# Attention outputs of two heads in the column halves of the array, and the first layer's input rows in that order

## The chip, the core and the metric
The kernel runs as one program on one core of a Trainium2 chip. The metric is the device time of one execution in microseconds (us). TensorE (PE) multiplies, and its weight loads are listed apart (PEld); VectorE (DVE), ScalarE (ACT) and GpSimd (POOL) do elementwise work; SyncE (SP) only issues transfers, and ScalarE issues some too. The engines run their own instruction streams in order and meet at semaphores.

## The reference
Three steps, in float32:

```
S[t] = a[t] * S[t-1] + k[t] v[t]^T      (a complex, |a| clipped to 0.999; batch 4, 8 heads, 768 steps, head size 48)
y[t] = q[t] . Re S[t]                   -> x: 3072 rows (batch x time) of 384 (heads x 48)
h = x @ w_in;  x2 = (h * clip(h + 3, 0, 6) / 6) @ w_out        (384 -> 2048 -> 384)
h = x2 @ w_in2; out = (max(h, 0) + alpha * min(h, 0)) @ w_out2 (384 -> 2048 -> 384)
```

## The kernel before
**Attention.** Time is cut into 24 chunks of 128 steps (six per batch). For a chunk, VectorE and ScalarE work out decay and phase of all heads (square root, arctangent, sine on ScalarE; reciprocals, running products and sums on VectorE), and multiply them into q and k (`prod`). Transfers from SyncE (`stack`, lines 328 to 338) and ScalarE (line 505) stack real and imaginary part of each head on 96 partitions (`st`). TensorE then forms the scores of four heads at a time (`score`, line 959), transposes k (`turn_k`, 968), and after VectorE's causal mask (719) the outputs (`outputs`, 971 to 984) and the new state (`new_state`, 990). These matmuls are in plain float32, each shown as two records. A batch's first chunk has no state yet, its last makes none.

**Outputs before.** The 384 rows of x are heads x 48, and they must lie on 3 blocks of 128 partitions. A head crosses a block's edge twice, so `head_tiles` lists 10 (head, block) pairs. Each is one matmul with 128 output columns, whose weights are a window of a zero-padded v (`v_pad`, 1536 columns) that puts the head's 48 columns at the right place; 10 more with `s_pad` add the state's part. ScalarE copies the result rounded (`x_high`, 516) and VectorE the rest (`x_low`, 725) into `x_hi` and `x_lo`.

**The two layers.** 8 units of 384 rows of x (three chunks each), 16 items a unit, 128 items a layer. An item is `hidden(n)`: 9 matmuls of 384 columns in float32r (three row blocks, each high x high, high x low, low x high), a gate on ScalarE and VectorE, a split into two parts (ScalarE line 528, POOL 439), and `output(n)`: 9 more. `output(n)` and `hidden(n + 3)` follow each other on TensorE.

**The order.** It is written out in `places()`. Slots run from -3 to 24; slots 0, 1, 2 have chunks 0, 1, 2, slot 3 has none, slots 4 to 24 have chunks 3 to 23. Each slot has positions 0 to 4 or more, one item to a position. While chunk c0 is at the scores, c1 and c2, the two behind it, are prepared on VectorE and ScalarE. TensorE does scores at position 0, outputs and state at 1; VectorE does `phases` and `mask` at 0, the products at 1, `x_low` and the state at 2, reciprocals at 3 and 4. SyncE's queue at position 2: the stacking of c1 (six transfers, then two), the loads of `a` (c0 + 4) and of `qk`; at position 3 the load of `v` for the next chunk. The items start at slot 3: 4, 4, 3, 5 in slots 3 to 6, then 5, 5, 6 in turn; after the 24 chunks 112 of the first layer's 128 items are done. `hidden(16u)`, the first of a unit, needs the whole unit's x and waits for `x_done` (line 1003).

**Weights.** `load_w` (317 to 326) brings the first layer's input weights in six transfers of 512 KB, each one row block of 128 and half of the columns; ScalarE's `split_w` (535 to 538) rounds 512 columns at a time, in order of row blocks, from slot -2 on, one to a position and ahead of that position's later work in its stream. In slot -2 the square root of chunk 0 (481) stands behind the first split.

A branch for inputs with too strong a decay follows the main program; it isn't entered here, and of its buffers only the place changes.

Of the kernel before, what the change touches and what calls it, by code (L numbers as in the profile page):

```python
# [16 lines left out]
P = 128  # L17
# [10 lines left out]
PADW = HD + P  # L28
PADTOT = P + HEADS * PADW
# [20 lines left out]

N1 = UNITS * MT_FF
# [28 lines left out]

def items_of(s):
    if s in ITEMS:
        before = sum(count for t, count in ITEMS.items() if t < s)
        return list(range(before, before + ITEMS[s]))
    if s <= CPU:
        return []
    u, j = divmod(s - 1, CPU)
    return list(range((u - 1) * MT_FF + MT_FF * j // CPU, (u - 1) * MT_FF + MT_FF * (j + 1) // CPU))
# [40 lines left out]
def build(nc, a_in, qk_in, v_in, w1_in, w1_out, w2_in, w2_out, alpha, x2_dram, out):  # L129
    with ExitStack() as ctx:  # L130
# [12 lines left out]
        x_hi = sb("x_hi", [P, 2, KT_DM, UT], F32R)  # L143
        x_lo = sb("x_lo", [P, 2, KT_DM, UT], F32R)
# [24 lines left out]
        v_pad = sb("v_pad", [P, PADTOT], F32, room)  # L169
        s_pad = sb("s_pad", [ROWS2, PADTOT], F32, room)  # L170
# [20 lines left out]
        y_blk = sb("y_blk", [P, KT_DM, BLK], F32, general)  # L191
        w_in_t = sb("w_in_t", [P, KT_DM, P], F32, general)
# [15 lines left out]
        yp3 = yp[:, 0:KT_DM * CH].rearrange("p (k t) -> p k t", k=KT_DM)  # L208
# [8 lines left out]
        wa_landed = [sem(f"wa_landed{i}") for i in range(10)]  # L217
# [74 lines left out]
        def _(sp):  # L292
# [24 lines left out]

            def load_w(n):
                if n < 6:
                    k, half_k = divmod(n, 2)  # L320
                    cols = slice(half_k * W_DMA, (half_k + 1) * W_DMA)
                    src = w1_in[k * P:(k + 1) * P, cols]
                    sp.dma_start(wa_raw[:, k * FF + cols.start:k * FF + cols.stop], src).then_inc(wa_landed[n], 16)
                else:
                    m0, m1 = 4 * (n - 6), 4 * (n - 5)
                    sp.dma_start(wb_raw[:, m0 * DM:m1 * DM].rearrange("p (m d) -> p m d", d=DM),
                                 w1_out[m0 * P:m1 * P, :].rearrange("(m p) d -> p m d", p=P)
                                 ).then_inc(wa_landed[n], 16)
# [25 lines left out]
            for w in range(6):  # L354
                load_w(w)
            for s, pos, n, c0, c1, c2, c3 in places():
                if pos == 2:
                    if c1 is not None:
                        stack(c1)
                    c4 = chunk_at(s + 4)  # L360
                    if c4 is not None and c4 >= 2:
                        load_a(c4)
                    if c2 is not None and c2 >= 1:
                        load_qk(c2)
# [7 lines left out]
                if n is not None and n % MT_FF == MT_FF - 1:  # L372
# [7 lines left out]
                         w2_in.rearrange("(k p) f -> p k f", p=P)).then_inc(w2i_landed, 16)  # L380
            load_x2(0)
# [53 lines left out]
        def _(pool):  # L435
# [12 lines left out]
            pool.memset(v_pad[:, :], 0.0).then_inc(pads_set, 1)  # L448
            pool.memset(s_pad[:, :], 0.0).then_inc(pads_set, 1)
# [16 lines left out]
            for n in range(N1 - MT_FF, 2 * N1 - GSTEP):  # L466
# [3 lines left out]
        def _(act):  # L470
# [41 lines left out]
            def x_high(c):  # L512
# [3 lines left out]
                act.activation(x_hi[:, u % 2, :, x_cols(c)], yp3, ACT.Copy).then_inc(xhi_done, 1)  # L516
# [599 lines left out]
```

## Time and profile before
| | us |
|---|---|
| time, median of 3 runs (lowest, highest) | 1083.95 (1082.51, 1084.04) |
| the profiled execution's time | 1083.26 |
| its span, first to last instruction | 1081.5 |
| TensorE busy in the span | 1009.7 (93%) |
| VectorE busy | 703.4 (65%) |
| ScalarE busy | 487.5 (45%) |
| mean granted TensorE clock | 0.981 |

Busy times are of the profiled execution. A matmul's end is modelled, so that neighbouring records overlap; the distance between two starts is the time that one takes in a stream. The granted clock is the share of full speed that TensorE was given: 1.00 is 2.4 GHz, 0.50 is 1.2 GHz. "[5.64 <-DVE gated L747]" behind a row says that the engine sat idle 5.64 us before it and what ended that. Rows of SPq are the issues of transfers in SyncE's queue, not the transfers. Slot starts are given by the first score matmul of the slot: 163.80 us is slot 6, then 187.42, 209.17, 233.24, 260.38, 284.46, 308.49 (slot 12), and 576.75 is slot 23.

### The profile page before, as it was taken

What the parts mean: (1) busy time and instruction counts of PE and PEld (TensorE: products, weight loads), DVE (VectorE), ACT (ScalarE), POOL (GpSimd) and SP (SyncE); (2) the same over time, 40 slices, a digit from 0 to 9 for tenths busy, and PEclk for the clock granted to TensorE, in tenths of its full rate; (3) what the DMA queues carried; (4) which work ended last, traced back from release to release, by engine and by line L of the source; (5) the groups of instructions that cost most, each with busy time, mean ns of one, the idle gap of its engine ahead of it and who ended that gap; (6) DMA issues with size and microseconds to landing.
All of it is one profiled execution on the core that took longest, in us unless ns stands there. A gap on an engine that the chain in (4) does not pass through costs nothing.

```text
span 1081.5 us, 16917 instructions
## 1 busy us (share of the span) xinstructions
PE 1009.7 (93%) x6354; PEld 1005.0 (93%) x6354; DVE 703.4 (65%) x1234; ACT 487.5 (45%) x814; POOL 305.8 (28%) x291
## 2 busy tenths in 40 slices
PE   0477789999999999999999999999999999999998
PEld 0477789999999999999999999999999999999997
DVE  4966999998998988889988234553433434343332
ACT  4644765676656666667664244331212212122221
POOL 3213421222222222222122233333333233333332
PEclk9968999999999999999999999999999999999999
DMA  5451233323233333232222070100101010101000
GB/s 182 132 147 30 67 95 99 94 67 88 68 77 102 87 87 89 67 89 67 70 74 74 13 277 1 45 24 22 45 1 44 1 45 1 44 1 45 1 22 23
DMA packets 77858, 70.47 MB, mean 65 GB/s; under 512 B 32592, under 2 KB 73552, under 8 KB 77392
## 3 DMA queue, kind: packets, MB, share of 16 engines
q1 hardware_dynamic: 68176, 61.07, 19.4%
q10 hardware_dynamic: 9600, 8.33, 2.9%
q8 instruction: 50, 0.82, 0.3%
q14 instruction: 32, 0.26, 0.1%
HBM read 40.90 MB, written 9.44 MB: 47 GB/s over the span
## 4 chain that ended last, share of the span: by engine, by line
PE 86%; DVE 7%; issue 2%; ACT 2%; SPq 1%; DMA 1%; ACTq 0%; DVEq 0%
PE op L995 12%; PE op L997 12%; PE op L996 12%; PE hp L997 12%; PE hp L995 12%; PE hp L996 12%; PE yp L980 5%; PE yp L983 4%; PE gp L990 2%; PE gp L959 2%; PE yp L959 2%; DVE t_inv L649 1%; PE tp L968 1%; DVE t_phase L665 1%; SPq L335 1%
## 5 line engine op out<-in xcount | busy, mean ns | idle before, releaser
L439 POOL TENSOR_TENSOR g_lo<-gated,g_hi 128x384 fp32r<-128x384 f32 x256 | 269.5, 1053 | 697.4 <-ACT g_hi L528 697.3
L528 ACT ACTIVATE g_hi<-gated 128x384 fp32r<-128x384 f32 x256 | 133.5, 522 | 357.5 <-DVE gated L761 291.4
L757 DVE TENSOR_SCALAR gate<-hp,alpha_sb 128x384 f32<-128x384 f32 x128 | 79.1, 618 | 230.5 <-PE hp L997 230.5
L995 PE MATMUL op<-g_hi,wb_hi 128*128 128x384 f32 x384 | 135.4, 353 | 2.3 <-POOL g_lo L439 2.3
L995 PE MATMUL hp<-x_hi,wa_hi 128*128 128x384 f32 x384 | 131.1, 341 | 6.1 <-DVE gated L747 6.1
L521 ACT ACTIVATE gate<-hp,half 128x384 f32<-128x384 f32 x128 | 73.7, 576 | 126.8 <-PE hp L997 115.0
L995 PE MATMUL op<-g_hi,wa_hi 128*128 128x384 f32 x384 | 129.9, 338 | 0.7 <-issue 0.7
L996 PE MATMUL op<-g_lo,wb_hi 128*128 128x384 f32 x384 | 130.0, 338 | 0.0
L997 PE MATMUL op<-g_hi,wb_lo 128*128 128x384 f32 x384 | 129.9, 338 | 0.0
L997 PE MATMUL op<-g_hi,wa_lo 128*128 128x384 f32 x384 | 129.8, 338 | 0.0
L997 PE MATMUL hp<-x_hi,w2i_lo 128*128 128x384 f32 x384 | 129.5, 337 | 0.0
L997 PE MATMUL hp<-x_hi,wa_lo 128*128 128x384 f32 x384 | 129.2, 337 | 0.0
L996 PE MATMUL hp<-x_lo,w2i_hi 128*128 128x384 f32 x384 | 129.2, 336 | 0.0
L995 PE MATMUL hp<-x_hi,w2i_hi 128*128 128x384 f32 x384 | 129.0, 336 | 0.0
L996 PE MATMUL hp<-x_lo,wa_hi 128*128 128x384 f32 x384 | 129.0, 336 | 0.0
L996 PE MATMUL op<-g_lo,wa_hi 128*128 128x384 f32 x384 | 128.8, 335 | 0.0
L747 DVE SCALAR_TENSOR_TENSOR gated<-gate,hp 128x384 f32<-128x384 f32 x128 | 70.0, 548 | 72.7 <-ACT gate L521 71.4
L980 PE MATMUL yp<-scores,v_pad 128*128 128x128 f32 x480 | 91.5, 286 | 3.5 <-DVE scores L719 3.3
L959 PE MATMUL gp<-st 96*128 96x128 f32 x192 | 29.3, 302 | 54.0 <-DMA st<-prod 54.0
L980 PEld LDWEIGHTS yp<-scores,v_pad 128*128 128x128 f32 x480 | 75.2, 202 | 4.4 <-DVE scores L719 4.4
L983 PE MATMUL yp<-st,s_pad 96*128 96x128 f32 x400 | 79.2, 280 | 0.0
L995 PEld LDWEIGHTS hp<-x_hi,wa_hi 128*128 128x128 f32 x384 | 72.6, 189 | 6.7 <-DVE gated L747 6.7
(97 smaller groups left out, 1978.5 us busy)
## 6 DMA issues: line engine op xcount, KB each, us to landing
st<-prod SPq DMA_DIRECT2D x48, 145.1 KB, 3.1
st<-prod ACTq DMA_DIRECT2D x48, 145.1 KB, 2.8
a_sb<-a_in SPq DMA_DIRECT2D x24, 288.0 KB, 3.5
qk_sb<-qk_in SPq DMA_DIRECT2D x24, 288.0 KB, 3.5
v_pad<-v_in SPq DMA_DIRECT2D x24, 192.0 KB, 3.2
x<-out_sb SPq DMA_DIRECT2D x8, 576.0 KB, 2.8
x_raw<-x SPq DMA_DIRECT2D x8, 576.0 KB, 4.6
out<-out_sb SPq DMA_DIRECT2D x8, 576.0 KB, 3.1
```

Source lines behind the costliest of these rows:

```text
L439: pool.tensor_tensor(g_lo[:, at, :], gated[:, at * UT:(at + 1) * UT], g_hi[:, at, :].bitcast(F32), ALU.subtract).then_inc(glo_done, 1)
L521: act.activation(gate[:, n % 2 * UT:(n % 2 + 1) * UT], hp[:, n % 2, 0:UT], ACT.Relu, bias=half[:, 0:1], scale=1.0 / 6.0).then_inc(gate_don ...
L528: act.activation(g_hi[:, at, :], gated[:, at * UT:(at + 1) * UT], ACT.Copy).then_inc(ghi_done, 1)
L747: dve.scalar_tensor_tensor(out=gated[:, to], in0=gate[:, at], scalar=1.0, in1=hp[:, n % 2, 0:UT], op0=ALU.min, op1=ALU.mult).then_inc(gate ...
L757: dve.tensor_scalar(gate[:, at], hp[:, n % 2, 0:UT], 0.0, alpha_sb[:, m:m + 1], ALU.min, ALU.mult).then_inc(gate_done, 1)
L959: mm = pe.matmul(score_banks[k][:, h % G4, :], st[:, c % 2, h, 1, 0:CH], st[:, c % 2, h, 0, 0:CH], start=True, stop=True)
L980: mm = pe.matmul(yp3[:, j, :], v_pad[:, cols], scores[:, h, :], start=(i == 0), stop=(is_first(c) and ends))
L983: mm = pe.matmul(yp3[:, j, :], s_pad[:, cols], st[:, c % 2, h, 0, 0:CH], start=False, stop=ends)
L990: mm = pe.matmul(kvp[:, h, :], k_rows[:, h, :], v_pad[:, P + h * PADW:P + h * PADW + HD], start=True, stop=True)
L995: pe.matmul(acc, lhs[0], rhs[0], start=start, stop=False)
L996: pe.matmul(acc, lhs[0], rhs[1], start=False, stop=False)
L997: return pe.matmul(acc, lhs[1], rhs[0], start=False, stop=stop)
```

## The change
- **Layout of x.** A pair of heads (2p, 2p + 1) takes one matmul region of 128 partitions: the even head on partitions 0 to 47, the odd on 64 to 111, with 16 unused partitions behind each. Four pairs would be four blocks; the layers still use three. So pairs 0 to 2 stay where they are, and the last pair's 2 x 48 rows are cut into 2 x 3 parts of 16 rows and moved into the unused partitions of blocks 0 to 2 (`spread`). `x_hi` and `x_lo` become one tensor `x_parts` with four blocks, of which the layers read three.
- **Outputs.** `v_pad` and `s_pad` hold 64 columns a head (48 and 16 zeros). A matmul has 64 output columns and writes partitions 0 to 63 for an even head and 64 to 127 for an odd one. Per pair the order is value part of the even and of the odd head, then state part of both: 8 and 8 matmuls a chunk for 10 and 10. The evictions to `x_hi` and `x_lo` cover four blocks of 128 columns for three.
- **Spread.** Six transfers within the on-chip memory per chunk, each 16 partitions x 2 (high, low) x 128 columns, issued by SyncE at position 2 behind the stacking of the next chunk and before the loads of `a` and `qk`. `hidden(16u)` waits for them instead of for `x_done`.
- **Input weights.** Their rows follow the new order: two halves of the columns, four transfers each (48, 16, 48 and 16 partitions, three row blocks in each). A split waits for all four of its half.
- **Items.** 3, 4, 3, 4 in slots 3 to 6, then 5, 5, 6 in turn; 110 are done when the chunks end, and the loop behind them begins at 110. SyncE stores unit 6 behind the load of the second layer's input weights.

```diff
-W_LOADS = {-1: range(6, 8), 0: range(8, 10)}
+W_LOADS = {-1: range(0, 2), 0: range(2, 4)}
-ITEMS = {CPU: 4, CPU + 1: 4, CPU + 2: 3, CPU + 3: 5}
+ITEMS = {CPU: 3, CPU + 1: 4, CPU + 2: 3, CPU + 3: 4}
...
-        x_hi = sb("x_hi", [P, 2, KT_DM, UT], F32R)
-        x_lo = sb("x_lo", [P, 2, KT_DM, UT], F32R)
+        x_parts = sb("x_parts", [P, 2, 2, PAIRS, UT], F32R)
+        x_hi, x_lo = x_parts[:, 0, :, :, :], x_parts[:, 1, :, :, :]
-        v_pad = sb("v_pad", [P, PADTOT], F32, room)
-        s_pad = sb("s_pad", [ROWS2, PADTOT], F32, room)
+        v_pad = sb("v_pad", [P, HEADS, HALF], F32, room)
+        s_pad = sb("s_pad", [ROWS2, HEADS, HALF], F32, room)
...
+            def load_w1(n):
+                cols = slice(n * W_DMA, (n + 1) * W_DMA)
+                to = wa_raw[:, :].rearrange("p (k f) -> p k f", f=FF)[:, :, cols]
+                low = w1_in[0:2 * KT_DM * HD, cols].rearrange("(k r d) f -> r d k f", r=2, d=HD)
+                high = w1_in[2 * KT_DM * HD:DM, cols].rearrange("(r k i) f -> r i k f", r=2, i=SPARE)
+                for r in range(2):
+                    at = r * HALF
+                    sp.dma_start(to[at:at + HD, :, :], low[r, :, :, :]).then_inc(wa_landed[n], 16)
+                    sp.dma_start(to[at + HD:at + HALF, :, :], high[r, :, :, :]).then_inc(wa_landed[n], 16)
...
+            def spread(c):
+
+                par = c // CPU % 2
+                sp.wait_ge(x_done, c + 1)
+                for r in range(2):
+                    for k in range(KT_DM):
+                        rows = slice(r * HALF + k * SPARE, r * HALF + (k + 1) * SPARE)
+                        to = slice(r * HALF + HD, (r + 1) * HALF)
+                        sp.dma_start(x_parts[to, :, par, k, x_cols(c)].bitcast(F32),
+                                     x_parts[rows, :, par, KT_DM, x_cols(c)].bitcast(F32)).then_inc(x_spread[par], 16)
...
                 if pos == 2:
                     if c1 is not None:
                         stack(c1)
+                    if c0 is not None:
+                        spread(c0)
...
-                act.activation(x_hi[:, u % 2, :, x_cols(c)], yp3, ACT.Copy).then_inc(xhi_done, 1)
+                act.activation(x_hi[:, u % 2, :, x_cols(c)], yp4, ACT.Copy).then_inc(xhi_done, 1)
...
-                act.wait_ge(wa_landed[n // 2 if n < NWI else 6 + (n - NWI) // 3], 16)
+                if n < NWI:
+                    act.wait_ge(wa_landed[n * WPC % FF // W_DMA], 16 * 4)
+                else:
+                    act.wait_ge(wb_landed[(n - NWI) // 3], 16)
...
-                for j, heads in enumerate(tiles):
-                    for i, (h, row) in enumerate(heads):
-                        cols = slice(P + h * PADW - row, P + h * PADW - row + P)
-                        ends = i == len(heads) - 1
-                        mm = pe.matmul(yp3[:, j, :], v_pad[:, cols], scores[:, h, :], start=(i == 0),
-                                       stop=(is_first(c) and ends))
-                        if not is_first(c):
-                            mm = pe.matmul(yp3[:, j, :], s_pad[:, cols], st[:, c % 2, h, 0, 0:CH], start=False,
-                                           stop=ends)
+                for p in range(PAIRS):
+                    for h in (2 * p, 2 * p + 1):
+                        at = h % 2 * HALF
+                        mm = pe.matmul(yp4[at:at + HALF, p, :], v_pad[:, h, :], scores[:, h, :], start=True,
+                                       stop=is_first(c))
+                    if not is_first(c):
+                        for h in (2 * p, 2 * p + 1):
+                            at = h % 2 * HALF
+                            mm = pe.matmul(yp4[at:at + HALF, p, :], s_pad[:, h, :], st[:, c % 2, h, 0, 0:CH],
+                                           start=False, stop=True)
...
-                    pe.wait_ge(x_done, (u + 1) * CPU)
+                    pe.wait_ge(x_spread[u % 2], 16 * SPREAD_DMAS * CPU * (u // 2 + 1))
...
-            for n in range(N1 - MT_FF, 2 * N1):
+            for n in range(N_ATT, 2 * N1):
```

## Rows read from the trace of the kernel before
**Rows 1.** The page's sections 1 and 5: busy us (share of the span) xinstructions; costliest groups.
```profile
PE 1009.7 (93%) x6354; PEld 1005.0 (93%) x6354; DVE 703.4 (65%) x1234; ACT 487.5 (45%) x814; POOL 305.8 (28%) x291
...
L980 PEld LDWEIGHTS yp<-scores,v_pad 128*128 128x128 f32 x480 | 75.2, 202 | 4.4 <-DVE scores L719 4.4
```
**Rows 2.** Windows, one per slot (6 to 10, 12, 23), then one of the second layer.
```profile
core 0: us, PE busy (x) PEld busy (x) DVE busy (x) ACT busy (x) POOL busy (x), PEclk, DMA share, GB/s
163.80:187.42 23.62, 23.62 (x146) 23.62 (x147) 21.86 (x39) 12.77 (x23) 5.36 (x5) 0.93 0.37 93
187.42:209.17 21.75, 21.75 (x151) 21.71 (x151) 20.17 (x38) 14.36 (x24) 4.41 (x4) 1.00 0.33 96
209.17:233.24 24.07, 24.07 (x171) 24.05 (x171) 23.16 (x41) 16.40 (x28) 6.25 (x6) 1.00 0.35 94
233.24:260.38 27.14, 27.14 (x189) 27.10 (x189) 23.44 (x42) 17.27 (x28) 6.15 (x6) 1.00 0.32 82
260.38:284.46 24.08, 24.08 (x171) 24.05 (x171) 20.91 (x38) 15.21 (x26) 5.36 (x6) 1.00 0.30 89
...
308.49:333.55 25.06, 25.06 (x165) 25.06 (x165) 22.42 (x40) 15.81 (x26) 5.68 (x6) 1.00 0.29 74
...
576.75:600.78 24.03, 24.03 (x172) 23.99 (x172) 15.76 (x30) 11.61 (x20) 5.24 (x5) 1.00 0.18 43
...
700.00:900.00 200.00, 200.00 (x1143) 200.00 (x1142) 83.27 (x138) 44.00 (x77) 65.88 (x64) 1.00 0.07 24
```
**Rows 3.** TensorE in order of time, slot 16: outputs, state, next item (start, us, what).
```profile
415.36 0.38 PE L980 MATMUL yp<-scores,v_pad 128*128 128x128 f32 x2
...
419.82 1.48 PE L990 MATMUL gp<-v_pad,k_rows 128*96 128x48 f32 x16
421.12 0.43 PE L995 MATMUL op<-g_hi,wb_hi 128*128 128x384 f32 x1
```
**Rows 4.** The start: chain, ScalarE in time, landings of the six loads, one window.
```profile
6.81 5.38 DMA wa_raw<-w_in
...
12.21 0.63 ACT L538 ACTIVATE wa_hi<-wa_raw 128x512 fp32r<-128x512 f32 x1 [5.52 <-DMA wa_raw<-w_in]
...
DMA to landing us min/median/max: 5.4/7.0/8.6
...
10.00:12.00 2.00, 0.00 (x0) 0.00 (x0) 0.00 (x0) 0.00 (x0) 0.00 (x0) 1.00 1.01 371
```
**Rows 5.** SyncE's queue in order of time: stacking issues of slots 6, 9, 12.
```profile
177.43 5.12 SPq L335 DMA_DIRECT2D st<-prod  x6
...
246.65 4.30 SPq L335 DMA_DIRECT2D st<-prod  x6
250.99 1.28 SPq L338 DMA_DIRECT2D st<-prod  x2
...
321.76 4.34 SPq L335 DMA_DIRECT2D st<-prod  x6
```
**Rows 6.** Transfer issues by group: KB each, median us from issue to landing.
```profile
v_pad<-v_in SPq DMA_DIRECT2D x24, 192.0 KB, 3.2
...
st<-prod SPq DMA_DIRECT2D x72, 16.1 KB, 2.4
```
**Rows 7.** VectorE's groups by shape: busy, mean ns | idle before, releaser.
```profile
L719 DVE TENSOR_TENSOR scores<-gp,causal 128x512 f32<-128x512 f32 x24 | 16.4, 684 | 2.0 <-PE gp L959 2.0
...
L725 DVE TENSOR_TENSOR x_lo<-yp,x_hi 128x384 fp32r<-128x384 f32 x24 | 13.2, 552 | 11.4 <-ACT x_hi L516 11.3
```
**Rows 8.** Slots 1 to 3 in order of time: SyncE, TensorE, and one window.
```profile
74.11 0.61 SPq L316 DMA_DIRECT2D v_pad<-v_in  x1
...
78.75 0.80 PE L980 MATMUL yp<-scores,v_pad 128*128 128x128 f32 x2
...
86.29 0.44 PE L995 MATMUL hp<-x_hi,wa_hi 128*128 128x384 f32 x1
...
95.32 0.69 PE L995 MATMUL hp<-x_hi,wa_hi 128*128 128x384 f32 x1 [5.64 <-DVE gated L747]
...
95.30:99.30 4.00, 3.98 (x12) 3.98 (x13) 0.51 (x2) 1.66 (x4) 1.98 (x2) 0.50 0.13 29
```

More of the change, by code:

```diff
@@ L27 @@
 WSZ = KT_DM * FF
-PADW = HD + P
-PADTOT = P + HEADS * PADW
+HALF = P // 2
 G4 = 4
@@ L49 @@
 STACK_DMAS = 2 * (2 + len(HIGH_PARTS))
+SPARE = HALF - HD
+SPREAD_DMAS = 2 * KT_DM
 N1 = UNITS * MT_FF
@@ L78, in chunk_at, with items_through @@
     return s - 1 if CPU < s <= NCH else None
+def items_through(s):
+    if s <= CPU + 3:
+        return sum(count for t, count in ITEMS.items() if t <= s)
+    return sum(ITEMS.values()) + (s - CPU - 3) * MT_FF // CPU
 def items_of(s):
[L82 to L88, printed above, removed]
+    return range(items_through(s - 1), items_through(s))
 def splits_at(s, pos):
@@ L103, in places @@
                    chunk_at(s + 3))
+N_ATT = items_through(NCH)
 def is_first(c):
@@ L116, in kept @@
     return c // CPB * (CPB - 1) + c % CPB
-def head_tiles():
-    return [[(h, h * HD - j * P) for h in range(HEADS) if h * HD < (j + 1) * P and (h + 1) * HD > j * P]
-            for j in range(KT_DM)]
 def need(eng, semaphore, count):
@@ L191, in build @@
         y_blk = sb("y_blk", [P, KT_DM, BLK], F32, general)
+        general.close()
+        general = ExitStack()
         w_in_t = sb("w_in_t", [P, KT_DM, P], F32, general)
@@ L216, in build @@
         qk_landed, v_landed = sem("qk_landed"), sem("v_landed")
-        wa_landed = [sem(f"wa_landed{i}") for i in range(10)]
+        wa_landed = [sem(f"wa_landed{i}") for i in range(2)]
+        wb_landed = [sem(f"wb_landed{i}") for i in range(4)]
+        x_spread = [sem(f"x_spread{i}") for i in range(2)]
         alpha_landed, raw_landed, x2_landed = sem("alpha_landed"), sem("raw_landed"), sem("x2_landed")
@@ L316, in load_v @@
                 sp.dma_start(win(v_pad), v_in[c, :, :].rearrange("t (h e) -> t h e", h=HEADS)).then_inc(v_landed, 16)
-            def load_w(n):
[L319 to L328, printed above, removed]
+            def load_w1(n):
[7 more added lines that the diff above has]
+                    sp.dma_start(to[at + HD:at + HALF, :, :], high[r, :, :, :]).then_inc(wa_landed[n], 16)
+            def load_w(n):
+                sp.dma_start(wb_raw[:, n * 4 * DM:(n + 1) * 4 * DM].rearrange("p (m d) -> p m d", d=DM),
+                             w1_out[n * 4 * P:(n + 1) * 4 * P, :].rearrange("(m p) d -> p m d", p=P)
+                             ).then_inc(wb_landed[n], 16)
+            def spread(c):
[7 more added lines that the diff above has]
+                                     x_parts[rows, :, par, KT_DM, x_cols(c)].bitcast(F32)).then_inc(x_spread[par], 16)
             def stack(c):
@@ L353, in _ @@
             load_v(0)
-            for w in range(6):
-                load_w(w)
+            for w in range(2):
+                load_w1(w)
             for s, pos, n, c0, c1, c2, c3 in places():
@@ L380, in _ @@
                          w2_in.rearrange("(k p) f -> p k f", p=P)).then_inc(w2i_landed, 16)
+            store_x2(UNITS - 2)
             load_x2(0)
@@ L465, in _ @@
                         low(k)
-            for n in range(N1 - MT_FF, 2 * N1 - GSTEP):
+            for n in range(N_ATT, 2 * N1 - GSTEP):
                 low(n + GSTEP)
@@ L598, in _ @@
                     split_x2(u + 1 - UNITS)
+                if m == MT_FF - 1:
+                    leave(u)
                 if n == N1 - 1:
-                    leave(u)
                     for k in range(2):
                         split_w2o(k)
-                if n >= N1 and m == MT_FF - 1:
-                    leave(u)
                 if u == UNITS:
@@ L824, in _ @@
                         gate1(k)
-            for n in range(N1 - MT_FF, 2 * N1):
+            for n in range(N_ATT, 2 * N1):
                 u, m = divmod(n, MT_FF)
@@ L949, in _ @@
         def _(pe):
-            tiles = head_tiles()
             def score(c, k):
@@ L989, in new_state @@
                 for h in range(HEADS):
-                    mm = pe.matmul(kvp[:, h, :], k_rows[:, h, :], v_pad[:, P + h * PADW:P + h * PADW + HD],
+                    mm = pe.matmul(kvp[:, h, :], k_rows[:, h, :], v_pad[:, h, 0:HD],
                                    start=True, stop=True)
@@ L1053, in _ @@
                         hidden(k)
-            for n in range(N1 - MT_FF, 2 * N1):
+            for n in range(N_ATT, 2 * N1):
                 output(n)
@@ L1057, in _ @@
                     hidden(n + HSTEP)
-                if n == N1 - MT_FF:
+                if n == N_ATT:
                     pe.wait_ge(bad_found, 1)
```

17 lines of the change are left out of this document (9 added, 8 removed).

## The prediction
> **What bounds the kernel now.** I read the page's first section, then the windows cut at each chunk's first score matmul, then the order of instructions on single engines, and last the chain at the start. The page gives TensorE 93% of the span and VectorE 65% [rows 1]. The windows say where that holds: from the chunk of slot 6 (163.80 us) on TensorE is busy for the whole of every slot, so a slot lasts as long as its matmuls [rows 2]. But VectorE is close behind. In slot 8 (209.17 to 233.24) it is busy 23.16 of 24.07 us, in slots 7, 9, 10 and 12 it is 20.17, 23.44, 20.91 and 22.42 of 21.75, 27.14, 24.08 and 25.06. After the chunks VectorE is far below (83.27 of 200 us in the last row). Before slot 6 TensorE idles and the chain runs through VectorE, ScalarE and transfers; it begins with a weight load: ScalarE stands at its first weight split until 12.21, where the chain has "DMA wa_raw<-w_in" from 6.81 for 5.38 us [rows 4]. The square root of chunk 0, on which all of VectorE's work waits, is queued behind that split.
>
> **Part 1, the output matmuls.** A later chunk has 10 value and 10 state matmuls, from 415.36 to the next kind at 419.82: 4.46 us, 0.223 us each (two records each) [rows 3]. After: 8 and 8, with 64 output columns, alternating between the halves. No row shows such a tile. Bounds: run one after another at the old price they save 4 x 0.223 = 0.89 us a chunk (0.45 where the chunk is a batch's first, 10 to 8); run two at a time they take 8 x 0.223 = 1.79 and save 2.68 (first: 1.34). The nearest row that shows what fewer columns do is the state update behind them: 48 moving columns against 96 weight columns, 16 records in 421.12 - 419.82 = 1.30 us, 0.081 each against 0.112 for 128 against 128 [rows 3]; so a record isn't a fixed price, and 64 weight columns leave room for two loads in the time of one. I take two at a time. Entering and leaving the half shape I put at 0.3 us a chunk, an estimate: each time about the part of a record that overlaps its neighbour (0.38 us for two records that are 0.22 apart [rows 3]), at most twice 0.16; lower end 0. Net 2.4 us (first 1.0), with ends 0.6 and 2.7.
>
> The Trainium skill, "TensorEngine Tiling (Array Packing)", section "Key Properties", says that different tiles can load weights and multiply in parallel, and that changing the tiling mode drains the engine. By the first half of that rule the chunk's outputs take 1.79 us, by the second they cost something on top; no row here shows either.
> The same skill, "TensorE: Matmul & The Clock Gate", Part 3, says that a weight load overlaps with a running matmul only where the row group differs. The two halves here share all rows, so this speaks for the serial rival below. The trace of now disagrees for whole tiles: records of the output matmuls come 0.112 us apart [rows 3] with a load of 0.202 us each [rows 1], which must overlap.
>
> **Part 2, the slots behind it.** TensorE's gain counts only until something else ends a slot.
> VectorE: its evictions of the outputs grow from 384 to 512 columns, 0.55 towards the 0.68 us of a 512-column one [rows 7], +0.13 a slot. With some 0.7 us that it can't avoid (in slot 8 it is idle 0.9 in all [rows 2]) a slot can't be shorter than its busy time + 0.8: 21.0 in slot 7, 24.0 in 8, 24.3 in 9, 21.7 in 10, 22.7 in 11 (busy some 21.9: slot 10's and one POOL-blocked operation more), 23.3 in 12.
> The spreading transfers: six per chunk on SyncE, behind the eight stacking issues of the next chunk. Slot 9: stacking from 246.65, its last two from 250.99 for 1.28, free at 252.3 [rows 5]; six issues of 0.6 = 3.6; the last lands 1.8 us after its issue ends, as the 16 KB stacking transfers do (2.4 from the start of the issue [rows 6]): 257.7. A unit's first hidden group (n = 16u), which is TensorE's last work of slots 6, 9, 12, ..., now waits for this. It takes 1.6 us (9 of the 0.175 us matmuls, 200 us / 1143 [rows 2]), so slot 9 can't end before 259.3, 26.0 after its start at 233.24. Slot 12: stacking from 321.76, 13.3 us after its start against 13.4 in slot 9, so 26.0 as well, against 25.06 now. Slot 6: stacking from 177.43 for 5.12, two more for 1.2, spread landed 189.2, group done 190.8: 27.0 us after 163.80, against 23.62 now.
> So, with TensorE's own limit (now - 2.4, first - 1.0): slot 6 +3.4; slot 7 20.7 against VectorE's 21.0, -0.75; slot 8 VectorE, -0.1; slot 9 the spread, -1.1; slot 10 VectorE, -2.4; slot 11 VectorE, -1.3; slot 12 the spread, +0.9. A cycle of six: -4.75; I take -4.3, since VectorE carries a lag from slot 8 into 9 and from 11 into 12. Slots 7 to 18 are two cycles, -8.6. Slots 19 to 24: -0.75, -0.1, -1.1, -2.4, then -2.4 twice, since VectorE has little left (15.76 of 24.03 in the last but one [rows 2]) and in slot 24 no stacking stands before the spread: -9.15.
>
> **Part 3, the items moved.** Slots 3 and 6 lose an item each; 110 instead of 112 are done when the chunks end. Two items of 18 matmuls of 0.175 us come back at the end, where TensorE alone counts: +6.3 us. In slot 6 the item's absence is in the 27.0 already. In slot 3 TensorE isn't the bound, and what goes from the chain is one gate on VectorE (0.55) and ScalarE's part: -1.0 (ends 0 and -3.1).
>
> **Part 4, the start.** The first split now needs half of all columns of all three row blocks: three times 512 KB, in four transfers. Six landings run from 12.2 to 18.5 us (issues 6.81 to 9.9, 5.4 to 8.6 to landing [rows 4]), 1.26 us per 512 KB, while the engines are full (share 1.01, 371 GB/s [rows 4]). Three lands at 14.7: +2.5 us on the chain that runs on to slot 6, lower end 0, upper end +6.3 if it landed with the last. The third split waits for the other half, about 18.5 to 19; the arctangent behind it isn't wanted before 20.8 + 2.5, so nothing more. The shorter clears on POOL hide behind SyncE's queue: v isn't issued before 6.16.
>
> **Part 5, slots 1 to 3.** The six spreading issues stand before the load of v: in slot 1 its issue moves from 74.11 to 77.7, lands 3.2 later at 80.9 [rows 6], and the outputs that began at 78.75 [rows 8] wait 2.1 us. Against that they get shorter: from 78.75 to the first hidden group at 86.29 [rows 8] are 7.5 us, 1.3 of them the state update, so 6.2 for 20 matmuls; with the halves in parallel (8 of 20) and the change of shape 2.9, so x is ready at 80.9 + 2.9 + 1.3 = 85.1. The first hidden group waits 3.6 + 1.8 us more for the spread, to 90.5. That isn't all lost: now the third group stands until 95.32 for VectorE's gate and then runs at a granted clock of 0.50, 1.2 GHz, at 0.32 us a matmul after 5.64 idle us, to 98.2 [rows 8]; the idle stretch moves ahead of the first group. Three groups of nine from 90.5, the first at 0.32 us (2.9), the second on the way up (2.4), the third at 0.175 (1.6), end at 97.4: -0.8. Serially (5.0 us for the outputs) all is 2.1 later: +1.3. From slot 4 on v has a reserve of some 6 us and nothing waits.
>
> **The sum.** +2.5 - 0.8 - 1.0 (to slot 6) + 3.4 (slot 6) - 8.6 - 9.15 + 6.3 = -7.3 us. From the profiled execution's 1083.26 (span 1081.5 + 1.8) that is 1076.0; its distance to the median of 1083.95 is 0.7, so 1076.7, say 1077.
>
> **The rivals.**
> B, serial halves: the array works through them one after another. For it: no row shows two tiles at once. Against: the record price follows the columns [rows 3], and the two halves write different partitions. Slot 6 +3.4; a cycle -0.15 -0.1 -0.6 x 3 + 0.9 = -1.15, two -2.3; the last six -0.15 -0.1 -0.6 x 4 = -2.65; the start 2.5 + 1.3 - 1.0 = +2.8; items +6.3. Sum +7.6: 1091.5, slower. Its price is the standing for the spread in slots 6, 12 and 18 and the two items, which a small saving doesn't pay; on the line between the two sums a net saving of 1.5 us a chunk breaks even.
> C, halves in parallel and the spread never late, because SyncE's stacking comes sooner or the transfers land sooner. For: SyncE idles much. Against: the stacking waits for VectorE's products, and that time is in [rows 5]. Slot 6 ends by VectorE, 21.86 - 0.55 + 0.8 = 22.1, -1.5; slots 9 and 12 -2.4 and -1.8, a cycle -8.75, two -17.5; the last six -10.45; -1.5 + 0.7 + 6.3 with these: -22.4, so 1061.5.
> D, in between: the halves overlap in part (a net saving near 1.5 us a chunk), or serial halves with a punctual spread (start +2.8, slot 6 -1.5, three sixes of -2.65, +6.3: -0.4). About 1084.
>
> **Chances.** Forecast 0.43, C 0.14, B 0.26, D 0.17. A measurement of this kernel tells 0.2% (2.2 us) from no change. D splits into 0.04 faster, 0.09 same, 0.04 slower; the forecast's lower part gives 0.04 to same. Faster 0.57, same 0.13, slower 0.30. Range 1064 to 1092; the forecast's own 1070 to 1082.
>
> **What would show it.** Output matmuls of a later chunk in 1.8 to 2.1 us (serial: 3.6), and a first matmul behind them that starts late by the change of shape; the chain with ScalarE waiting for wa_raw until 14.7; TensorE idle 5 to 9 us before the group of n = 16 in slot 6, and 1 to 3 us at the end of slots 9, 12, 15, 18, 21; slot 8 as long as now, with VectorE without a gap; 110 items done at the last chunk's end and 6.3 us more behind it. The forecast is wrong if a chunk's outputs take over 3 us, if TensorE doesn't wait in slot 6, or if the first split starts after 17.

## The result and the profile after

| | before | after |
|---|---|---|
| time, median (lowest, highest), us | 1083.99 (1082.51, 1084.67), 4 runs | 1095.51 (1091.72, 1096.93), 4 runs |
| profiled execution: time, span | 1083.26, 1081.5 | 1091.72, 1089.9 |
| TensorE busy | 1009.7 (93%) | 971.5 (89%) |
| first score matmul | 36.33 | 48.86 |
| start of slot 6 | 163.80 | 174.21 |
| start of slot 24 | 600.78 | 605.67 |

The changed kernel is slower: ratio 1.0103, 95% interval 1.0074 to 1.0131. The forecast was 1077 in a range of 1064 to 1092. TensorE is busy 38 us less and the kernel takes 11.5 us longer. The profiled execution is the quickest of the four, 3.8 us below their median, so the trace accounts for 8.4 of the 11.5 us.

The page of the kernel after, sections 1 and 5 (the answers to [rows 1] and two groups that are new):
```profile
PE 971.5 (89%) x6178; PEld 952.6 (87%) x6178; DVE 700.0 (64%) x1234; ACT 487.9 (45%) x814; POOL 304.5 (28%) x291
...
L1023 PE MATMUL hp<-x_parts,wa_hi 128*128 128x384 f32 x384 | 133.9, 349 | 19.4 <-DMA x_parts<-x_parts 18.0
L1023 PE MATMUL op<-g_hi,wb_hi 128*128 128x384 f32 x384 | 136.7, 356 | 9.4 <-ACT out_sb L559 8.6
```
The last figures are TensorE's idle time ahead of a group: 18.0 us of waits for the spread, and 8.6 us for ScalarE's copy of a finished unit, which stood nowhere before.

The start of the kernel after (chain, ScalarE, the eight landings), for [rows 4]:
```profile
10.70 19.48 DMA wa_raw<-w_in
...
21.00 0.63 ACT L567 ACTIVATE wa_hi<-wa_raw 128x512 fp32r<-128x512 f32 x1 [14.57 <-DMA wa_raw<-w_in]
...
DMA to landing us min/median/max: 7.3/13.6/19.5
```
The first split starts 8.8 us later than before, and the third, at 30.20 (10.70 + 19.48, where the chain's transfer ends), holds up the next chunk's squares and, behind them, chunk 0's arctangent (33.29 us for 20.76), so the first scores are 12.5 us late.

TensorE in slot 17 of the kernel after, for [rows 3]:
```profile
451.55 0.44 PE L1006 MATMUL yp<-scores,v_pad 128*64 128x128 f32 x4
451.82 0.39 PE L1011 MATMUL yp<-st,s_pad 96*64 96x128 f32 x4
...
453.14 0.39 PE L1011 MATMUL yp<-st,s_pad 96*64 96x128 f32 x4
453.46 1.56 PE L1018 MATMUL gp<-v_pad,k_rows 128*96 128x48 f32 x16
454.84 0.42 PE L1023 MATMUL op<-g_hi,wb_hi 128*128 128x384 f32 x1
```
Four records, two matmuls on two halves, take the 0.22 us that one matmul took. The outputs last 1.91 us for 4.46. The state update behind them takes 1.38 for 1.30.

SyncE and TensorE in slot 6 of the kernel after, for [rows 5]:
```profile
188.37 4.23 SPq L358 DMA_DIRECT2D st<-prod  x6
192.64 1.23 SPq L361 DMA_DIRECT2D st<-prod  x2
193.91 3.83 SPq L350 DMA_DIRECT2D x_parts<-x_parts  x6
...
199.02 0.69 PE L1023 MATMUL hp<-x_parts,wa_hi 128*128 128x384 f32 x1 [7.46 <-DMA x_parts<-x_parts]
```
Windows of the kernel after, slots 6 to 10, 12, 13, 15, 19 and 23, then the second layer, for [rows 2]:
```profile
core 0: us, PE busy (x) PEld busy (x) DVE busy (x) ACT busy (x) POOL busy (x), PEclk, DMA share, GB/s
174.21:201.99 27.78, 19.76 (x120) 18.98 (x121) 22.50 (x40) 12.28 (x20) 4.29 (x4) 0.82 0.37 94
201.99:226.41 24.42, 22.50 (x147) 21.92 (x147) 20.78 (x37) 16.20 (x26) 5.55 (x5) 0.93 0.29 77
226.41:248.07 21.66, 21.66 (x164) 21.21 (x164) 20.61 (x39) 13.97 (x24) 4.23 (x4) 1.00 0.33 86
248.07:274.18 26.11, 25.04 (x182) 24.24 (x182) 24.23 (x43) 17.06 (x29) 6.54 (x7) 1.00 0.35 89
274.18:297.04 22.86, 21.86 (x163) 21.28 (x163) 20.46 (x38) 15.96 (x26) 5.74 (x6) 1.00 0.34 91
...
319.62:345.44 25.82, 23.54 (x157) 22.14 (x157) 22.79 (x40) 15.51 (x26) 6.06 (x7) 1.00 0.33 89
345.44:369.86 24.42, 22.49 (x148) 21.90 (x148) 20.78 (x37) 16.20 (x26) 6.02 (x6) 0.93 0.32 87
...
391.51:419.72 28.21, 26.33 (x182) 25.54 (x182) 24.24 (x43) 17.07 (x29) 7.25 (x7) 0.95 0.37 93
...
490.43:513.28 22.85, 20.91 (x148) 20.33 (x148) 20.35 (x37) 15.96 (x26) 5.84 (x6) 1.00 0.34 90
...
584.05:605.67 21.62, 21.62 (x163) 21.16 (x163) 16.05 (x30) 11.62 (x20) 5.11 (x6) 1.00 0.29 70
...
700.00:900.00 200.00, 200.00 (x1144) 200.00 (x1143) 83.95 (x139) 45.17 (x80) 66.64 (x64) 1.00 0.07 25
```
In numbers (us a slot, from the starts of the score matmuls):

| slot | before | forecast | after |
|---|---|---|---|
| 6 | 23.62 | 27.0 | 27.78 |
| 7 | 21.75 | 21.0 | 24.42 |
| 8 | 24.07 | 24.0 | 21.66 |
| 9 | 27.14 | 26.0 | 26.11 |
| 10 | 24.08 | 21.7 | 22.86 |
| 11 | 24.03 | 22.7 | 22.58 |
| 12 | 25.06 | 26.0 | 25.82 |

The reader is to see three things: TensorE is no longer busy for the whole slot; the slots where it is (8 and 23) are 2.4 us shorter, as forecast for the outputs; and slot 7, in which the last item of a unit stands, is 2.7 us longer than before, which no step of the forecast has.

The windows show one thing more. Slots 7, 13 and 15 have a granted clock of 0.93, 0.93 and 0.95, while in the kernel before every slot from 7 to 23 has 1.00. In each of them TensorE waits once, for 1.92, 1.93 and 1.88 us, and behind that wait its matmuls of 384 columns start 0.32 us apart instead of 0.175, for some 3 to 4.5 us: the clock is at 1.2 GHz instead of 2.4. Slot 19 has the same work as slot 13 and a wait of 1.94 us, but its clock stayed at 1.00, and it lasts 22.85 us for 24.42. So a wait of 1.9 us costs 1.9 us in one slot and 3.5 in another.

### The profile page after: what moved, and what is told of

The parts are those of the page before. It is cut to its first block, busy times and chain, and to the rows that moved or that the text cites. A ratio compares the mean times of both kernels' runs of the same rounds, so it can differ in the third digit from the quotient of the medians.

```text
span 1089.9 us, 16711 instructions
## 1 busy us (share of the span) xinstructions
PE 971.5 (89%) x6178; PEld 952.6 (87%) x6178; DVE 700.0 (64%) x1234; ACT 487.9 (45%) x814; POOL 304.5 (28%) x291
## 4 chain that ended last, share of the span: by engine, by line
PE 55%; DVE 19%; ACT 8%; SPq 7%; issue 6%; DMA 4%; ACTq 1%; DVEq 0%
PE hp L1023 9%; PE op L1023 9%; PE hp L1025 9%; PE hp L1024 9%; PE op L1025 9%; PE op L1024 8%; SPq L358 3%; DVE t_phase L693 3%; DVE t_fb L728 3%; SPq L350 2%; ACT L515 2%; DMA wa_raw<-w_in 2%; DVE scores L747 2%; DVE t_inv L677 2%; DVE gated L775 2%
## 5 line engine op out<-in xcount | busy, mean ns | idle before, releaser
L1023 PE MATMUL hp<-x_parts,wa_hi 128*128 128x384 f32 x384 | 133.9, 349 | 19.4 <-DMA x_parts<-x_parts 18.0
L1024 PE MATMUL hp<-x_parts,wa_hi 128*128 128x384 f32 x384 | 130.9, 341 | 0.0
L1025 PE MATMUL hp<-x_parts,wa_lo 128*128 128x384 f32 x384 | 130.6, 340 | 0.0
L1025 PE MATMUL hp<-x_parts,w2i_lo 128*128 128x384 f32 x384 | 129.5, 337 | 0.0
L1024 PE MATMUL hp<-x_parts,w2i_hi 128*128 128x384 f32 x384 | 129.2, 336 | 0.0
L1023 PE MATMUL hp<-x_parts,w2i_hi 128*128 128x384 f32 x384 | 129.0, 336 | 0.0
L1023 PEld LDWEIGHTS hp<-x_parts,wa_hi 128*128 128x128 f32 x384 | 73.9, 192 | 22.5 <-DMA x_parts<-x_parts 20.1
L986 PEld LDWEIGHTS gp<-st 96*128 96x128 f32 x192 | 28.7, 220 | 73.7 <-DMA st<-prod 73.7
L1023 PEld LDWEIGHTS op<-g_hi,wb_hi 128*128 128x128 f32 x384 | 73.7, 192 | 12.0 <-ACT out_sb L559 9.3
L789 DVE SCALAR_TENSOR_TENSOR gated<-hp,gate 128x384 f32<-128x384 f32 x128 | 71.4, 558 | 4.4
```

Source lines behind the costliest of these rows:

```text
L789: dve.scalar_tensor_tensor(out=gated[:, to], in0=hp[:, n % 2, 0:UT], scalar=0.0, in1=gate[:, at], op0=ALU.max, op1=ALU.add).then_inc(gated ...
L986: mm = pe.matmul(score_banks[k][:, h % G4, :], st[:, c % 2, h, 1, 0:CH], st[:, c % 2, h, 0, 0:CH], start=True, stop=True)
L1023: pe.matmul(acc, lhs[0], rhs[0], start=start, stop=False)
L1024: pe.matmul(acc, lhs[0], rhs[1], start=False, stop=False)
L1025: return pe.matmul(acc, lhs[1], rhs[0], start=False, stop=stop)
```

## The experiments

**1 and 2. The eight loads alone, away and added.** Edit of the first, on the changed kernel (the second puts the changed `load_w1` and its waits into the kernel before). The copy of the weights in the new row order is laid out ahead of the launch, like the kernel's other inputs:
```diff
-                low = w1_in[0:2 * KT_DM * HD, cols].rearrange("(k r d) f -> r d k f", r=2, d=HD)
-                high = w1_in[2 * KT_DM * HD:DM, cols].rearrange("(r k i) f -> r i k f", r=2, i=SPARE)
...
+                src = w1_rows[k * P:(k + 1) * P, cols]
+                sp.dma_start(wa_raw[:, k * FF + cols.start:k * FF + cols.stop], src).then_inc(wa_landed[n], 16)
...
-                    act.wait_ge(wa_landed[n * WPC % FF // W_DMA], 16 * 4)
+                    act.wait_ge(wa_landed[n // 2], 16)
```


> The changed kernel, with the first layer's input weights taken from a copy whose rows already lie in the new order, by the six loads of 512 KB of the kernel before and with their waits; all else as changed. Theory (the eight loads in 48 and 16 partitions are slow and cost the start): the first weight split starts at 12.2 us again instead of 21.0, the first score matmul at 36.4 instead of 48.9, and the time falls by the 12 us, to 1083 to 1084. Rival (the start is late because SyncE and the spreading stand in the way, the loads are slow only in their last part): first score after 42, time over 1088.

Measured: 1080.49 us, ratio 0.9974 (0.9963 to 0.9985) to the kernel before. First split at 12.31, first score at 36.44, slot 6 at 160.88. Without the eight loads the change is a small gain, 15.0 us below the changed kernel; the expectation of 1083 to 1084 was 3 us too high. From slot 6 to slot 24 the two traces are alike (430.95 us for 431.46).

> The kernel before, with only the eight loads of the change in place of its six and the wait of a split for the four loads of its half of the columns; the rows of the weights then lie in an order that this kernel's x doesn't have, so the result is another. Theory: first split at 21, first score at 48 to 49, time 1084 + 10 to 12.5 = 1094 to 1096.5. Rival (the loads cost little by themselves): 1084 + 2.5 = 1086.5.

Measured: 1096.52 us, ratio 1.0119 (1.01 to 1.0139), 12.4 us more than the kernel before in the same series; first split 20.97, first score 49.70. The loads cost the same in a kernel that has nothing else of the change. The rival, 1086.5, falls.

**3. The wait for half of the columns.** Six loads of 128 partitions, in the order of the halves:
```diff
+                for k in range(KT_DM):
+                    src = w1_rows[k * P:(k + 1) * P, cols]
+                    sp.dma_start(wa_raw[:, k * FF + cols.start:k * FF + cols.stop], src).then_inc(wa_landed[n], 16)
...
+                act.wait_ge(wa_landed[n * WPC % FF // W_DMA], 16 * KT_DM)
```


> The changed kernel with rows in the new order in memory, six loads of 128 partitions x 1024 columns, but in the order of the halves (three row blocks of the first half, then of the second), and a split waits for all three of its half, as in the change. It tells the wait for a whole half from the slowness of the loads. Theory (slowness): first split at 14.7 us, 2.5 later than in the kernel before, first score at 39. Rival (the wait is what costs): first split near 21.

**4 and 5. Destination or source.** On the changed kernel; first the destinations of the change with rows as they lie, then one load for all partitions:
```diff
+                src = w1_in[:, cols].rearrange("(k p) f -> p k f", p=P)
+                for at, rows in ((0, HD), (HD, SPARE), (HALF, HD), (HALF + HD, SPARE)):
+                    sp.dma_start(to[at:at + rows, :, :], src[at:at + rows, :, :]).then_inc(wa_landed[n], 16)
```
```diff
+                sp.dma_start(to, w1_in[:, cols].rearrange("(k p) f -> p k f", p=P)).then_inc(wa_landed[n], 16)
```


> The changed kernel; the eight weight loads keep their partitions (48, 16, 48, 16, three row blocks in each) but read rows as they lie (row k x 128 + p for partition p), so that only the destination's narrowness is left of the change. The weights' rows then don't fit x. Theory (few partitions at a time make a load slow): first split at 20 to 21 us as in the changed kernel. Rival (the memory side: which rows one load reads): 15.

> The changed kernel with two weight loads, each of one half of the columns for all 128 partitions and all three row blocks at once (rows as they lie, so the rows don't fit x). It keeps the three blocks in one load and takes the narrowness away. Theory (narrowness): the half lands when its bytes can, first split at 14.5 to 15.5 us. Rival (three row blocks in one load are what is slow): 20 to 21.

The first split of each on ScalarE (start, us, what): experiment 3, then 4, then 5.
```profile
15.35 0.63 ACT L563 ACTIVATE wa_hi<-wa_raw 128x512 fp32r<-128x512 f32 x1 [9.13 <-DMA wa_raw<-w_rows]
```
```profile
20.93 0.63 ACT L564 ACTIVATE wa_hi<-wa_raw 128x512 fp32r<-128x512 f32 x1 [14.81 <-DMA wa_raw<-w_in]
```
```profile
14.96 0.63 ACT L562 ACTIVATE wa_hi<-wa_raw 128x512 fp32r<-128x512 f32 x1 [8.73 <-DMA wa_raw<-w_in]
```
The same stretch of 8 us in the kernel before and in experiment 4 (columns as in the windows above; the last two are the transfer engines' busy share and GB/s):
```profile
12.00:20.00 8.00, 0.00 (x0) 0.00 (x0) 5.10 (x7) 6.52 (x9) 4.47 (x3) 1.00 0.87 319
```
```profile
12.00:20.00 8.00, 0.00 (x0) 0.00 (x0) 0.00 (x0) 0.00 (x0) 0.00 (x0) 1.00 1.02 165
```
The wait for a half costs 3 us (15.35 for 12.21; first score 39.41 for 36.33), which is the forecast's mechanism, for which it had 2.5. The other 5.6 us of the first split, and the late third, come with the loads of few partitions: rows as they lie change nothing (20.93 for 21.00), all partitions at once mend it (14.96). It isn't the number of loads either, since experiment 3 has three for a half of the columns and the change has four. In the stretch shown the transfer engines are fully busy at half the rate. Why loads of few partitions are slow the runs don't tell.

The times, one run each: 1087.02 us for experiment 3, 1096.60 for 4 and 1087.24 for 5. Experiments 3 and 5 thus lie 6.5 us above experiment 1, and not 3; the part on the prediction comes back to that.

**6. The spread away.**
```diff
-                    if c0 is not None:
-                        spread(c0)
...
-                    pe.wait_ge(x_spread[u % 2], 16 * SPREAD_DMAS * CPU * (u // 2 + 1))
+                    pe.wait_ge(x_done, (u + 1) * CPU)
```


> As the kernel with ordered rows and six loads, but without the spreading transfers: the first hidden group of a unit waits for VectorE's part of x alone. The last pair of heads is missing in the first layer's input. Theory (the spread ends slots 6, 9, 12, 15, 18, 21 and delays v): slot 6 falls from 27.8 to 20 to 23 us, slots 12 and 18 from 26 to 23, TensorE waits nowhere for x_parts; together 10 to 15 us less than with the spread, 1070. Rival (VectorE is the bound there anyway): 2 to 5 us less.

Measured: 1071.52 us, ratio 0.9888 (0.9869 to 0.9907), 9.0 us below experiment 1 in the same series. No wait for x_parts is left. Slot 6 is 20.55 us for 27.43, but slot 7 is 27.51 for 24.16: together -3.5. Slot 7 in this run:
```profile
179.04:206.55 27.51, 25.79 (x146) 25.21 (x147) 23.02 (x41) 16.06 (x27) 5.44 (x6) 0.82 0.41 110
```
TensorE is busy 25.79 of the 27.51 us there, at a granted clock of 0.82: twice, behind a wait for the stacked q and k (2.27 us) and behind one for the copy of a finished unit (1.72 us), its matmuls run at 1.2 GHz for 3 to 4 us. Slots 12 and 18 fall from 26.26 and 26.01 to 25.07 and 24.53. The size lies just under the theory's 10 to 15 and above the rival's 2 to 5; the waits for the copy of a unit grow from 8.4 us in all to 10.6, so that it is rather a lower bound of what the spread costs.

**7. The items of before, with the spread.**
```diff
-ITEMS = {CPU: 3, CPU + 1: 4, CPU + 2: 3, CPU + 3: 4}
+ITEMS = {CPU: 4, CPU + 1: 4, CPU + 2: 3, CPU + 3: 5}
```


> As the kernel with ordered rows and six loads (1080.5 us), but with the items of the kernel before: 4, 4, 3, 5 in slots 3 to 6, 112 done at the end of the chunks. The first hidden group of a unit then stands two items earlier, where the spread hasn't landed. Theory: two items fewer behind the chunks (-6.3 us), but TensorE waits some 3 to 6 us more in slots 6, 9, 12, 15, 18, 21: 5 to 20 us slower in all. Rival: VectorE is the bound in the chunks, the waits cost nothing more, 1074 to 1078.

Measured: 1116.59 us, ratio 1.0302 (1.0285 to 1.0319), 36 us above experiment 1, more than the theory's 20. TensorE's waits (engine, what waited for what: us in total, times, longest):
```profile
PE hp L1018 <- DMA x_parts<-x_parts: 58.5, 8, 10.6
```
With these items TensorE waits 58.5 us for the spread, for 17.6 in experiment 1: the two items that the change moved behind the chunks (+6.3 us) buy off some 40 us of waits. No wait for a unit's copy is left here, which shows that it, too, came with the moved items.

**8. The copy of a finished unit, earlier.** On the kernel of experiment 1:
```diff
                 if pos == 1 and c1 is not None:
                     waves(c1)
+                if n is not None and n % MT_FF == MT_FF - 1:
+                    leave(n // MT_FF)
                 if pos == 2 and c0 is not None:
                     x_high(c0)
...
-                if n is not None and n % MT_FF == MT_FF - 1:
-                    leave(n // MT_FF)
```


> As the kernel with ordered rows and six loads, but ScalarE's copy of a finished unit out of the accumulators stands ahead of the first chunk work that follows the item's own (behind the sines, ahead of the k copy and the square root) instead of at the end of the position. The moved items put a unit's last item at position 1, with a long ScalarE queue behind it; in slots 7, 10, 13, 16, 19, 22 TensorE waited 0.8 to 1.9 us for that copy. Theory (this wait is a cost of the moved items): the waits on out_sb go, 4 to 8 us less than 1080.5. Rival (VectorE is the bound in those slots): the waits go and the time falls by under 2 us.

Measured: 1073.65 us, ratio 0.9902 (0.9886 to 0.9919), against 0.9974 in experiment 1: some 7 us. The waits on out_sb are gone. The six slots that had them are 8.1 us shorter in all, the most slot 13 with 21.73 us for 24.43, of which some 1.6 are the clock (1.00 for 0.93); slot 7 gives 1.1 (23.03 for 24.16). The other slots give back 3.9, the most slot 18 (28.48 for 26.01). This is ScalarE in slot 7 of the changed kernel, which shows why the copy was late:
```profile
211.84 1.28 ACT L507 ACT_TABLE_LOAD   x1
213.14 0.52 ACT L507 ACTIVATE t_mag<-t_sq 128x384 f32<-128x384 f32 x1
213.69 0.62 ACT L511 ACTIVATE t_ce<-t_mag,tiny 128x384 f32<-128x384 f32 x1
214.21 1.11 ACT L559 ACTIVATE out_sb<-op 128x1152 f32<-128x1152 f32 x1
```
With the items moved, a unit's last one stands at position 1, and the table load and the square root come ahead of its copy, while TensorE's next item waits 1.92 us for it.

**9. Neighbours on the same half.** On the kernel of experiment 1:
```diff
-                for p in range(PAIRS):
-                    for h in (2 * p, 2 * p + 1):
-                        at = h % 2 * HALF
+                for par in range(2):
+                    for p in range(PAIRS):
+                        h, at = 2 * p + par, par * HALF
```


> As the kernel with ordered rows and six loads, but the output matmuls in the order: all even heads (value, state, next pair), then all odd heads, so that neighbours in the stream use the same half of the array. Number, shapes and results are the same. Theory (two halves work at the same time only where neighbours in the stream are on different halves): a later chunk's outputs take 16 x 0.223 = 3.6 us instead of 1.9. Rival (a matmul of 64 columns is cheap by itself, the halves don't work side by side): 1.9 as before.

Measured: 1087.99 us in one run. TensorE's outputs in slot 18:
```profile
465.19 0.43 PE L1002 MATMUL yp<-scores,v_pad 128*64 128x128 f32 x2
465.45 0.38 PE L1005 MATMUL yp<-st,s_pad 96*64 96x128 f32 x2
465.68 0.38 PE L1002 MATMUL yp<-scores,v_pad 128*64 128x128 f32 x2
...
466.56 0.44 PE L1002 MATMUL yp<-scores,v_pad 128*64 128x128 f32 x4
466.78 0.44 PE L1005 MATMUL yp<-st,s_pad 96*64 96x128 f32 x4
467.05 0.38 PE L1002 MATMUL yp<-scores,v_pad 128*64 128x128 f32 x2
```
One matmul in 0.22 us again, 3.28 us in all for 1.91. Only at the seam, where the stream passes from the even to the odd heads (466.56), do two share the time. A row that writes another place than its neighbour (465.68 behind 465.45) takes 0.22 us as well, so it isn't the repeated place in the accumulator that costs. So the gain is work side by side, by the order in the stream; the cheap-matmul rival falls.

**10. The better kernel: SyncE's queue in another order.** On the kernel of experiment 8, and so with the weights' rows laid out ahead of the launch:
```diff
+                    last = c0 is not None and c0 % CPU == CPU - 1
                     if c1 is not None:
-                        stack(c1)
-                    if c0 is not None:
+                        stack(c1, c0 if last else None)
+                    elif last:
                         spread(c0)
...
+                    if c0 is not None and c0 % CPU < CPU - 1:
+                        spread(c0)
                     for w in W_LOADS.get(s, ()):
...
+                if ended is not None:
+                    spread(ended)
                 sp.wait_ge(prod_done, 2 * c + 2)
```


> As the kernel with ordered rows, six loads and the early copy of a finished unit (1073.7 us), with the spreading issues moved in SyncE's queue: for a unit's last chunk between the first six and the last two stacking transfers, for other chunks behind the load of v. Theory: the spread lands 1.2 us sooner where a unit waits for it and v isn't late any more (TensorE waited 4.4 and 2.8 us for it in slots 1 and 2), so 3 to 7 us less, 1067 to 1071. Rival (the stacking that now comes later ends the slot instead, or VectorE does): 1072 to 1075.

Measured: 1062.00 us (1061.96 to 1062.88), ratio 0.9803 (0.979 to 0.9817): 2.0% faster than the kernel before, and 11.6 us below experiment 8, more than the theory's 3 to 7. TensorE's waits:
```profile
PE hp L1024 <- DMA x_parts<-x_parts: 11.0, 2, 6.0
PE gp L1019 <- ACT k_rows L537: 5.9, 8, 1.4
```
The waits for v are gone, and slot 2 begins 1.5 us earlier than in experiment 8, slot 4 5.1 us (114.38 for 119.47), slot 6 5.7 us. The spread is waited for in slots 2 and 6 alone. Behind slot 6 another 7.4 us go, the most in slot 18 (25.10 for 28.48), then in slots 9, 7, 15, 11 and 21, with 1.0 to 1.5 each; from slot 7 to 23 the granted clock is 1.00, and two of experiment 8's slots were below that beside slot 7 (18 and 19, 0.96 and 0.98). How much of the 7.4 us is the clock and how much the queue, one trace of each doesn't tell.

**11. One item later still.**
```diff
-ITEMS = {CPU: 3, CPU + 1: 4, CPU + 2: 3, CPU + 3: 4}
+ITEMS = {CPU: 3, CPU + 1: 4, CPU + 2: 3, CPU + 3: 3}
```


> The same, with 3 instead of 4 items in slot 6: every later item is one further back, a unit's first hidden group stands at position 0 of the next slot behind the scores, and 109 items are done when the chunks end. Theory (a wait for the spread is worth moving out of the slot's end): the waits of 1 to 2 us in slots 9, 12, 15, 18, 21 go and slot 6 gets shorter by 1 to 3, one item more behind the chunks costs 3.1: within 3 us of the kernel beside it. Rival: the group at position 0 holds up VectorE's first gate of the slot, 5 us or more slower.

Measured: 1065.93 us, ratio 0.984 (0.9825 to 0.9856), 3.9 us slower than experiment 10, between the theory's 3 and the rival's 5. Slot 6 is 2.6 us shorter and slot 7 2.0 longer; the start of slot 24 is 1.2 us later in spite of an item less, and that item costs its 3.1 behind the chunks.

## Why the prediction was wrong

Forecast -7.3 us, trace +8.4, a miss of 15.7. Of its own three signs of being wrong one came true: the first split starts after 17. By its steps:

- **Part 4, the start: the step that failed.** +2.5 was the price of waiting for a half, and experiment 3 gives about 3 for it. "Three lands at 14.7" took 1.26 us per 512 KB from six loads of 128 partitions and applied it to loads of 48 and 16. They ran at 165 GB/s, and the split started at 21.0. "The third split waits for the other half, about 18.5 to 19 ... so nothing more" fell with it: 30.20. Together the start costs 12.5, beyond even the stated upper end of 6.3. This step carries 10 of the 15.7 us.
- **Part 1, outputs: right.** 1.91 us for 1.79, the state update 0.08 longer: the change of shape costs 0.2 us a chunk where 0.3 was taken. A chunk is 2.41 us shorter where TensorE sets the pace (slots 17, 23), forecast 2.4. Experiment 9 shows that the two halves work side by side. The Trainium skill, "TensorEngine Tiling (Array Packing)", section "Key Properties", says that different tiles can load weights and multiply in parallel; the trace agrees, with two matmuls in the 0.22 us of one. The Trainium skill, "TensorE: Matmul & The Clock Gate", Part 3, says that a weight load overlaps with running matmuls only where the row group differs; the trace disagrees: both halves use the same rows, their records start 0.055 us apart, and each has a load of 0.147 us:
```profile
L1006 PEld LDWEIGHTS yp<-scores,v_pad 128*64 128x64 f32 x384 | 25.4, 147 | 17.6 <-issue 15.2 <-DVE scores L747 2.5
```
- **Part 2, the spread: right in place, and in size but for the clock.** Slot 6 27.78 for 27.0, slot 9 26.11 for 26.0, slot 12 25.82 for 26.0. Experiments 6 and 7 show that it is this wait. In slot 6 the spread landed a little sooner than forecast (24.8 us after the slot's start for 25.4), but the nine matmuls behind the 7.46 us of waiting took 2.97 us for the forecast's 1.6, since most of them ran at 1.2 GHz. Slot 15, which was to be like slot 9, lasts 28.21: it waits 0.8 us longer (1.88 for 1.07) and is busy 1.3 longer at its lower clock.
- **Part 2, VectorE as the bound: wrong in slot 8.** "24.0 in 8" was its busy time in a window cut at TensorE's starts. In [rows 2] that window holds the operation of line 655 twice, at its beginning (that of the slot before) and near its end:
```profile
209.87 1.50 DVE L655 TENSOR_TENSOR t_dt<-t_dt,t_inv 128x768 f32<-128x768 f32 x1
...
232.45 1.50 DVE L655 TENSOR_TENSOR t_dt<-t_dt,t_inv 128x768 f32<-128x768 f32 x1
```
  The work of one slot is less: 21.66 us were possible, in slot 8 and likewise in 14 and 20. Over slots 7 to 12 the busy time fits (132.0 us before, 130.6 after), slot by slot it doesn't.
- **A step that was missing: the copy of a unit.** Part 3 moved items and counted only their own time. It didn't follow what stands at a unit's last item, ScalarE's copy out of the accumulators: TensorE waits 8.6 us for it in six slots (experiments 7 and 8).
- **A second one: the clock behind a wait.** Part 5 counted a low clock behind its waits; parts 2 and 3 took 0.175 us a matmul throughout. In slots 7, 13 and 15 the lower clock costs some 1.6, 1.6 and 1.3 us, an estimate from slot 19 (22.85 us for 24.42) and from slot 9 (busy 25.04 us for 26.33). Slots 7 and 13 are +2.7 instead of -0.75 by the wait and the clock together.
- **The sum behind slot 6 owes much to luck.** Slots 8, 14 and 20 gave 2.3 us each more than forecast, slots 7 and 13 3.4 less, slot 19 1.8 less and slot 15 2.2 less. So slots 7 to 12 came to -2.7 for -4.3, slots 13 to 18 to -1.2 for -4.3, slots 19 to 23 to -5.8 for -6.75.
- **Part 3, the two items: right.** From the start of slot 24 to the end +3.5, forecast 6.3 - 2.4 = 3.9.
- **Parts 3 and 5, the way to slot 6: right in the sum, not in its terms.** From the start of slot 0 to that of slot 6 the forecast had -1.8, the trace has -2.1. The wait for v in slot 2 is 2.31 us, forecast 2.1; one of 4.44 in slot 1 it didn't have. To the start of slot 4 the trace has -0.1; then slot 4 gives -2.6 and slot 5 +0.5, for which the forecast had nothing, and why slot 4 gets shorter no run tells. The late v cost more than it seemed: experiment 10 took 5.7 us off the way to slot 6.

The rival B had the right sign and nearly the right time, 1091.5, by luck: its halves were serial, and they weren't.

What remains is that the profiled execution lies 3.8 us below the median of the four. Their mean granted clocks were 0.986 (1091.72), 0.972 (1094.68), 0.979 (1096.33) and 0.971 (1096.93). There is one trace of these four, but experiment 3 has the same instructions behind the start. From slot 6 to slot 24 its trace is 435.36 us for 431.46, 3.9 longer, and TensorE is busy 408.4 us for 405.4 with the same matmuls. The difference lies most in slots 18, 19 and 22: 27.86, 24.63 and 24.43 us at a granted clock of 0.95, 0.91 and 0.93, for 26.13, 22.85 and 22.86 at 1.00. Slots 18 and 19 of experiment 3:
```profile
454.70:482.56 27.86, 25.14 (x157) 23.28 (x157) 23.84 (x41) 16.54 (x28) 7.42 (x7) 0.95 0.35 91
482.56:507.19 24.63, 22.93 (x148) 22.35 (x148) 20.75 (x37) 16.09 (x26) 5.72 (x5) 0.91 0.28 77
```
So which of the waits the clock falls behind differs from run to run, and between these two that makes 3.0 of the 3.9 us. It fits the spread of the four runs, and the place of experiment 3 above experiment 1; for those runs themselves it isn't shown. The kernel before has no such waits behind slot 6, and its four runs lie within 2.2 us.

## What to carry to other kernels

A transfer's time is not its bytes: before a load is cut into pieces with few partitions, look for a row with such a destination, and where there is none, put the worst case at half the rate. When items of a schedule are moved, list everything that hangs on particular items (first and last of a unit), and see what stands ahead of it in each engine's stream at the new place. Cut a second engine's windows at its own marks before you take its busy time as a bound. And a short wait in the middle of busy TensorE time can cost more than its length: read the granted clock behind it.

## What the runs showed of the hardware

- Loads from memory into 48 and 16 partitions, with 4 KB rows: 165 GB/s at a busy share of 1.02 (experiment 4), against 371 at 1.01 for 128 partitions [rows 4].
- Plain float32 matmuls with 64 output columns in alternating column halves: 0.11 us each in a stream, 0.22 each where neighbours use the same half; entering and leaving that shape cost about 0.2 us together.
- The granted clock behind waits of TensorE, kernel after: it fell to 1.2 GHz for 2 to 4.5 us behind waits of 1.88, 1.92, 1.93 and 7.46 us (slots 15, 7, 13, 6) and stayed at 2.4 behind one of 1.94 (slot 19); in experiment 3 it fell behind one of 1.00 (slot 22).
